# Moving a chunk's carried part and state in front of its values, in a fused mLSTM and two-layer feed-forward kernel

## The reference

```python
for t in range(S):                                  # attention, per batch and head
    m_new = np.maximum(f_gate[:, :, t] + m, i_gate[:, :, t])
    f_stab = np.exp(f_gate[:, :, t] + m - m_new)
    i_stab = np.exp(i_gate[:, :, t] - m_new)
    C = f_stab * C + i_stab * outer(v_t, k_t)
    n = f_stab * n + i_stab * k_t
    y[t] = sigmoid(o_t) * (C @ q_t) / max(abs(n . q_t), 1)
h = x @ w_in;  g = max(h, 0) + alpha * min(h, 0);  x1 = g @ w_out      # 320 -> 2048 -> 320
h = max(x1 @ w1, x1 @ w2, x1 @ w3);  out = h @ w_out2                   # 320 -> 768 -> 320
```

## Time and profile before

| | us |
|---|---|
| median of 3 runs | 748.95 (747.39 to 749.24) |
| the profiled execution | 748.46 |
| its span, first to last instruction | 746.7 |
| PE busy in it | 737.6 (99%) |
| DVE, ACT, POOL busy | 455.0, 306.9, 175.4 |
| mean granted TensorE clock | 0.998 of full |

### The profile page before, as it was taken

The page is one execution under the profiler, slowest core; times in us unless marked ns, Lnnn a source line. Parts: engine busy times, 40 slices in busy tenths (PEclk is TensorE's granted clock), DMA queues, the critical chain, the costliest instruction groups (busy, mean ns, idle before and its releaser), DMA issues.

```text
span 746.7 us, 11542 instructions
## 1 busy us (share of the span) xinstructions
PE 737.6 (99%) x4430; PEld 652.4 (87%) x4430; DVE 455.0 (61%) x774; ACT 306.9 (41%) x646; POOL 175.4 (23%) x201
## 2 busy tenths in 40 slices
PE   8899999999999999999999999999999999999998
PEld 6899999999988888888888888888888888888886
DVE  7787787799778868776877548633242424324232
ACT  6675744645564446444643446311212112121211
POOL 6697154164243324332431000000000000000000
PEclk9999999999999999999999999999999999999999
DMA  9973322423223213221200270030202002000101
GB/s 237 287 206 110 120 67 66 124 71 98 96 86 105 75 39 119 92 87 35 67 2 0 103 218 0 1 120 2 77 1 77 1 1 78 1 35 1 36 1 35
DMA packets 30407, 55.66 MB, mean 75 GB/s; under 512 B 3176, under 2 KB 19024, under 8 KB 29968
## 3 DMA queue, kind: packets, MB, share of 16 engines
q1 hardware_dynamic: 29888, 54.49, 23.8%
q10 hardware_dynamic: 464, 0.43, 0.2%
HBM read 46.96 MB, written 7.95 MB: 74 GB/s over the span
## 4 chain that ended last, share of the span: by engine, by line
PE 90%; DVE 4%; POOL 2%; issue 2%; ACT 2%; DMA 1%; SPq 0%; DVEq 0%; ACTq 0%; POOLq 0%
PE bank L794 26%; PE bank L757 22%; PE bank L680 6%; PE bank L772 6%; PE bank L774 5%; PE bank L773 5%; PE bank L809 3%; PE bank L810 3%; PE bank L811 3%; PE bank L776 3%; PE bank L777 3%; PE bank L688 2%; PE bank L696 1%; PE bank L718 1%; PE bank L730 1%
## 5 line engine op out<-in xcount | busy, mean ns | idle before, releaser
L757 PE MATMUL bank<-x_split,w_hi 128*128 128x512 f32 (+2 forms) x560 | 167.4, 366 | 2.0 <-ACT x_split L898 2.0
L757 PE MATMUL bank<-x_split,w_lo 128*128 128x512 f32 (+2 forms) x336 | 120.1, 360 | 0.0
L940 ACT ACTIVATE g_full<-bank 128x512 f32<-128x512 f32 (+2 forms) x112 | 59.8, 534 | 135.4 <-PE bank L757 134.4
L757 PEld LDWEIGHTS bank<-x_split,w_hi 128*128 128x128 f32 x560 | 102.6, 189 | 14.5 <-ACT x_split L898 2.2
L1184 DVE SCALAR_TENSOR_TENSOR g_full<-g_full,beta,bank 128x512 f32<-128x512 f32 (+2 forms) x112 | 74.6, 666 | 40.7 <-ACT g_full L940 40.1
L1165 DVE TENSOR_TENSOR g_lo<-g_full,g_hi 128x512 fp32r<-128x512 f32 (+2 forms) x112 | 79.5, 710 | 32.5 <-ACT g_hi L949 31.7
L1205 DVE TENSOR_TENSOR best<-bank,first_of_max 128x512 f32<-128x512 f32 x36 | 24.9, 692 | 102.5 <-PE bank L794 76.1
L772 PE MATMUL bank<-g_hi,wproj 128*128 128x512 f32 (+2 forms) x224 | 83.9, 374 | 0.8 <-DVE g_lo L1165 0.8
L949 ACT ACTIVATE g_hi<-g_full 128x512 fp32r<-128x512 f32 (+2 forms) x112 | 63.1, 564 | 48.1 <-DVE g_full L1184 47.9
L774 PE MATMUL bank<-g_hi,wproj 128*128 128x512 f32 (+2 forms) x224 | 80.5, 359 | 0.0
L773 PE MATMUL bank<-g_lo,wproj 128*128 128x512 f32 (+2 forms) x224 | 80.3, 358 | 0.0
(11 more groups left out here) (135 smaller groups left out, 1379.7 us busy)
## 6 DMA issues: line engine op xcount, KB each, us to landing
u_bcast<-u_scratch SPq DMA_DIRECT2D x21, 512.0 KB, 3.9
kv<-in_kv SPq DMA_DIRECT2D x24, 324.0 KB, 3.0
q_t<-in_q_t SPq DMA_DIRECT2D x24, 180.0 KB
k_t<-in_k_t SPq DMA_DIRECT2D x72, 60.0 KB
out<-final SPq DMA_DIRECT2D x5, 640.0 KB, 3.8
wproj_raw<-in_w_out SPq DMA_DIRECT2D x4, 640.0 KB, 11.1
o_gate<-in_o_gate SPq DMA_DIRECT2D x4, 640.0 KB, 4.5
w_raw<-in_w_max SPq DMA_DIRECT2D x2, 1152.0 KB, 6.4
```

Of the source, the lines that this page charges most:

```text
L757: ins = pe.matmul(ps[:, 0:cols], w[:, a, f], xs[:, x, 0:cols], start=(m == 0), stop=(m == 7))
L940: act.activation(gf[:, n % GF_SLOTS, 0:cols], hid[j % HID_BANKS][:, 0:cols], ACT.Relu, scale=-1.0).then_inc(neg_done, 1)
```

## The change

The six groups of a chunk stay six. The second group held "carry" (the carried part and the state, on PE and DVE), and now holds the first half of the next chunk's gate (ACT only); the third group held "values" and that half gate, and now holds "carry" and then "values". Nothing else is changed; the order of `TASKS` stays the same.

```diff
-    return [[("scores", ch)] + soon * [("prepare", ch + 1)], [("carry", ch)],
-            [("values", ch)] + more * [("gate", ch + 1, 0)],
+    return [[("scores", ch)] + soon * [("prepare", ch + 1)], more * [("gate", ch + 1, 0)],
+            [("carry", ch), ("values", ch)],
             more * [("gate", ch + 1, 1)] + [("finish", ch, 0)],
             [("finish", ch, 1)] + pack * [("pack", ch + 1, 0)] + later * [("prepare", ch + 2)],
             pack * [("pack", ch + 1, 1)]]
```

## The result

The changed kernel takes 777.73 us (median of 5 runs, 775.29 to 778.59) against 747.74 (5 runs of the kernel before beside it): a ratio of 1.0387, with a 95% interval of 1.0369 to 1.0405 (the two medians by themselves divide to 1.0401). The prediction was 772.5 us, range 765 to 779. The profiled execution took 778.06 us, with a span of 776.3 us, 29.6 more than before.

What follows compares the result with a forecast made beforehand. TensorE (PE), busy 737.6 of 746.7 us, was taken as the bound. Stalls of 20.3 us plus clock 5.4 less 1.8 saved gave +23.9 on 748.46, stated as 772.5 us, range 765 to 779.

Steps and rivals of the forecast that it cites:

- Three long stalls, 14.4 us: Chunks 8, 16, 20, behind H2 with the sigmoid before it: values1 waits 4.8 us each for DVE's carry-bank read.
- The clock, 5.4 us: Half clock behind the stalls: 1.7 us at each of chunks 8, 16 and 20, plus 0.3 at chunk 2.
- Block 0, 4.6 us of stalls: Half gate waits for POOL's mask; values1 stalls 2.7 us at chunk 2, 0.8 at 3, 1.1 at 4.
- Chunk 5, 0.5 us: Half gate between sigmoid and high part in short steps, P1 waiting for the low part: 0.5 us, between 0 and 1.
- Small stalls at chunks 15 and 19, 0.8 us: Behind a hidden step with nothing else in the way, values1 stalls 0.4 us at each of two chunks.
- Switches saved, 1.8 us: Joining two attention visits saves PE one 0.08 us return to layer 1 in each of 22 chunks.
- the one with a full clock: Rival: the clock holds at full behind the stalls, so 767 us; chance 0.2.
- The one of 779 us: Rival: delays feed on each other, seven chunks behind project steps stall 0.5 us each, half clock lasts longer; chance 0.12.

Runs made afterwards that it cites:

- filler run: Changed kernel plus 20 bfloat16 matmuls of 512 columns in front of values0 of chunks 8, 16 and 20, overwritten by it: 771.74 us.
- the run with block 0's gates late: Changed kernel, but for chunks 2, 3 and 4 the half gate stays behind the values: 769.88 us, ratio 1.0276 to the kernel before.
- the run with carry alone: Kernel before with carry and state moved in front of the values, both half gates left where they were: 757.89 us, ratio 1.0125.
- the gate alone: Kernel before with the first half gate moved into the second group behind carry, which stays there; values alone in the third: 756.22 us, ratio 1.0107.
- the clear chunks: Kernel before with the new order only for chunks 7, 9, 10, 11, 14, 17, 18, 21, 22, 23: 748.93 us against 748.99.

## Why the prediction was right

The direction and the time (777.7 in 765 to 779) came out, and the mechanism is the one that it named. Its reading of the earlier trace rows missed one ring wait of 0.3 us ahead of block 0, on which nothing hangs. By its terms:

- **Three long stalls, 14.4 us.** Measured 4.56, 4.60 and 4.61, together 13.8. Taking sigmoid and table loads out of the queue brought them to 1.0, so ACT's order makes 3.6 of the 4.6. What I had not seen is that the other 1.0 is not ACT's doing; by the timeline it is the scores' work on DVE two steps before.
- **The clock, 5.4 us.** Too small. The term was mis-sized in two places. Behind each long stall the shift of PE exceeds the wait by 2.2 to 2.6 us (chunk 8: 7.1 against 4.6), not 1.7; the half clock began in the wait and held on longer. The filler run gives 2.0 each. In the run with block 0's gates late the same three waits cost 1.7 each, just my figure, so that the excess does not lie in the length of the wait; what it lies in is open. And at chunk 2 I let chunk 3's wait for the mask absorb it and put 0.3, where the half clock behind the wait cost 3.4 us (some 6.8 us at half). It was not absorbed: chunk 3 waited for nothing, because PE came later than the mask. Chunk 2 shifted PE by 5.0 us: 3.2 of wait and 3.4 of clock, less the 1.7 us of the earlier trace rows that this kernel did not lose.
- **Block 0, 4.6 us of stalls.** Measured 3.2, 0.0 and 0.9, together 4.1, where I had 2.7, 0.8 and 1.1. The wait for the mask ended where I put it (39.2), POOL's decay waited 3.28 us for the state (3.2 predicted), and chunk 2's release came at 42.2. PE was there 0.5 us earlier than I took: the half clock of the earlier trace rows did not occur.
- **Chunk 5, 0.5 us.** Measured 1.4, in waits of PE for low parts of about 0.2 us at three projections and the slower starts around them. The carry step, moved away from between H1 and H2, had been cover for the low part of H0.
- **Small stalls at chunks 15 and 19, 0.8 us.** The waits were 0.13 each, and the steps behind them came some 0.3 us later; chunks 11 to 13 lost about 0.7 more that I had at zero.
- **Switches saved, 1.8 us.** This step failed. The shifts of PE across the undisturbed chunks (7, 9, 10, 17, 18) change by 0.02 to 0.04 us each, and the run with ten of them changed was equal to before. The rows say why: before, state's three matmuls took 0.58 us up to the hidden step and the 0.08 us gap came behind its first matmul; after, they take 0.67 us up to the values (297.75 to 298.42). Leaving float32 matmuls cost the same for both followers seen here, the hidden step's and the values'. I had named this as a bound and taken the wrong end.

Stalls 20.3 against 18.9 idle, clock 5.4 against 10.7 longer busy, saved 1.8 against none: the misses are in the clock and the switches, and both made the forecast 5 us too fast. Of the 10.7 us the clock rows give 9.1: 10.8 behind the waits (3.4 at chunk 2; 2.7, 2.4 and 2.2 at the long ones) less the 1.7 of the kernel before; the rest is slower starts. Part of the hit is luck. The range held with 1.3 us to spare, less than the 1.7 us which the changed kernel gained at the first hidden step, where the half clock of the earlier trace rows stayed away (in the profiled execution, and by the mean clock of 0.982 in all five runs in the others too); nothing in the forecast had counted on that. Of the rivals, the one with a full clock would have been 767 us; the filler run, at 771.7, is the nearest to it that was run. The one of 779 us was half right: the half clock did last longer, but of the chunks behind a project step of layer 1 in blocks 1 to 5 only chunk 10 waited for the carry bank, for 0.11 us.

## What to carry to other kernels

Work that is moved directly in front of its user loses the steps that hid its way back: ask which queue the answer comes through, and what stands in that queue at each place where the pattern repeats, since one pattern gave no wait above 0.11 us at ten chunks and 4.6 us at three. Two edits that lengthen the same chain do not add: 9 and 8 us alone became 30 together. A wait of an engine that is the bound costs more than its length when its clock falls behind it. Where such a wait can't be shortened, filling it is worth something: here 6.0 us for three waits, against 17.8 us for the run that took the sigmoid out of the queue and so shortened them. Splitting a wait was not tried.

## What the runs showed of the hardware

**The clock behind idle time.** Waits of 4.6 us were followed by half clock in all six cases (three in the changed kernel, three in the run with block 0's gates late), and the one of 3.2 us in the changed kernel was too. Of waits near 2 us some were and some were not: in the run with carry alone two of three, and at the first hidden step the kernel before showed it and the changed one did not, with 2.0 and 2.2 us of waiting. The cost did not follow the length of the wait: 1.7 us behind waits of 2.0 in the kernel before and with carry alone, about 3.1 behind waits of 2.3 at the first hidden step in the runs with the gate alone and with the clear chunks, 3.4 behind 3.2 us, and behind 4.6 us 2.2 to 2.6 in one kernel and 1.7 in another. The Trainium skill, page "TensorE: Matmul & The Clock Gate", section "HAM oscillation — how this bites in real kernels", has bursts of matmuls with waits of some 3 to 5 us between them each start at half rate; the trace agrees for the waits of 3.2 and 4.6 us, and shows that a wait near 2 us is sometimes followed by it and sometimes not.

**DVE beside POOL.** A DVE operation on 8 elements a partition took 0.17 us in the kernel before and 1.00 us while POOL made its mask (1.09 us); a low part of 384 columns took 0.56 us in the median of the kernel before, 1.02 in the rows above and 1.44 at most beside a mask, in the kernel before as well. The Trainium skill, page "SBUF — State Buffer", section "Who interferes with whom", has the two engines share a pair of ports that one of them holds for its whole instruction; the rows agree, in that the small operation ends with the mask, and not some per cent later than usual. Moving POOL's work away was worth 3.4 us where DVE was late, and nothing where it was not.
